# Weight pieces loaded to other places and earlier, x split by ScalarE and GpSimd, and the activation ahead of the mask

## What is computed

```python
def _attn_ref(q, k, v, tau):
    scores = scale * np.matmul(q, k.transpose(0, 1, 3, 2))
    thresh = np.max(scores, axis=-1, keepdims=True) - tau
    scores = np.where(scores >= thresh, scores, -1000000000.0)
    scores = scores - np.max(scores, axis=-1, keepdims=True)
    attn = np.exp(scores)
    attn = attn / (np.sum(attn, axis=-1, keepdims=True) + 1e-09)
    return np.matmul(attn, v)
def _moe_ref(x, w_in, w_out, alpha):        # 512 -> 2048 -> 512
    h = x @ w_in
    return (np.maximum(h, 0.0) + alpha * np.minimum(h, 0.0)) @ w_out
def _moe2_ref(x, w1, w2, w3, w_out):        # 512 -> 1024 -> 512
    return (((x @ w1) * (x @ w2)) @ w3) @ w_out
```

## Time and profile before

| | us |
|---|---|
| median of 3 timed runs | 1059.4 (1058.19 to 1060.02) |
| the profiled execution | 1060.03 |
| its span | 1058.1 |

### The profile page before, as it was taken

The page is one execution under the profiler, slowest core; times in us unless marked ns, Lnnn a source line. Parts: engine busy times, 40 slices in busy tenths (PEclk is TensorE's granted clock), DMA queues, the critical chain, the costliest instruction groups (busy, mean ns, idle before and its releaser), DMA issues.

```text
span 1058.1 us, 18205 instructions
## 1 busy us (share of the span) xinstructions
PE 990.3 (94%) x6848; PEld 899.6 (85%) x6848; DVE 519.6 (49%) x1374; ACT 420.0 (40%) x1000; POOL 472.2 (45%) x580
## 2 busy tenths in 40 slices
PE   3799956999999999999999999999999999999998
PEld 2566634777877787889999999999999999999998
DVE  6888977899998998922332222222111111111111
ACT  5666655666665666434323333333111111211210
POOL 5877768766666656323444444444212111111211
PEclk9799986999999999999999999999999999999999
DMA  7389898787878686768153222263211011011000
GB/s 261 86 242 276 263 302 199 197 229 185 234 196 237 184 208 181 198 168 300 56 198 131 113 112 113 112 250 133 91 68 45 24 68 46 23 68 46 24 23 24
DMA packets 53224, 156.39 MB, mean 148 GB/s; under 512 B 8208, under 2 KB 20496, under 8 KB 49424
## 3 DMA queue, kind: packets, MB, share of 16 engines
q1 hardware_dynamic: 42144, 122.78, 37.3%
q10 hardware_dynamic: 10992, 32.45, 10.8%
HBM read 79.05 MB, written 32.51 MB: 105 GB/s over the span
## 4 chain that ended last, share of the span: by engine, by line
PE 61%; DVE 13%; DMA 7%; POOL 5%; issue 5%; ACT 4%; SPq 4%; ACTq 1%; POOLq 0%
PE psum L693 19%; PE psum L726 19%; PE psum L679 11%; PE psum L638 5%; DVE nmx L940 5%; DMA zbuf<-ybuf 4%; DVE e_ring L953 4%; PE psum L600 3%; SPq L443 3%; POOL g L1069 2%; PE psum L651 2%; PE psum L583 2%; DVE g_raw L985 1%; ACT g_raw L840 1%; DMA k_raw<-k 1%
## 5 line engine op out<-in xcount | busy, mean ns | idle before, releaser
L1069 POOL TENSOR_TENSOR g<-g_raw,g 128x288 fp32r<-128x288 f32 x192 | 158.7, 831 | 378.8 <-ACT g L922 235.1
L726 PE MATMUL psum<-xy,w_a 128*128 128x288 f32 x1536 | 206.1, 295 | 0.6 <-DVE y_buf L1053 0.6
L726 PEld LDWEIGHTS psum<-xy,w_a 128*128 128x128 f32 x1536 | 205.2, 188 | 0.8 <-DVE y_buf L1053 0.8
L583 PE MATMUL psum<-ks,qs 128*128 128x288 f32 x640 | 121.4, 320 | 37.3 <-DVE e_ring L953 25.3
L583 PEld LDWEIGHTS psum<-ks,qs 128*128 128x128 f32 x640 | 101.2, 204 | 53.9 <-DVE e_ring L953 35.5
L1098 POOL TENSOR_SCALAR e_ring<-e_ring,rden,uni 128x576 f32<-128x576 f32 x144 | 118.6, 825 | 60.3 <-DVE rden L964 56.8
L805 ACT ACTIVATE e_ring<-psum,nmx 128x576 f32<-128x576 f32 x144 | 106.7, 741 | 82.1 <-DVE nmx L940 82.0
L985 DVE SCALAR_TENSOR_TENSOR g_raw<-g_raw,beta_sb,psum 128x288 f32<-128x288 f32 x128 | 65.7, 514 | 127.2 <-ACT g_raw L840 127.0
L953 DVE SCALAR_TENSOR_TENSOR e_ring<-psum,thr,e_ring 128x576 f32<-128x576 f32 x144 | 115.4, 801 | 12.4 <-ACT e_ring L805 11.9
L600 PE MATMUL psum<-zbuf,vs 128*64 128x320 f32 (+1 forms) x640 | 107.9, 433 | 13.7 <-DMA zbuf<-ybuf 10.9
L940 DVE TENSOR_REDUCE nmx<-psum 128x1 f32<-128x576 f32 x144 | 108.5, 753 | 22.7 <-PE psum L583 22.3
(11 more groups left out here) (53 smaller groups left out, 1105.7 us busy)
## 6 DMA issues: line engine op xcount, KB each, us to landing
zbuf<-ybuf SPq DMA_DIRECT2D x96, 180.0 KB, 4.4
raw_a<-weights SPq DMA_DIRECT2D x56, 256.0 KB, 6.9
zbuf<-ybuf SPq DMA_DIRECT2D x96, 144.0 KB, 4.3
xy<-xs SPq DMA_DIRECT2D x12, 1152.0 KB, 5.2
q_raw<-q ACTq DMA_DIRECT2D x16, 576.0 KB, 6.2
xs<-x_hl SPq DMA_DIRECT2D x32, 288.0 KB, 6.1
ys<-xy SPq DMA_DIRECT2D x8, 1152.0 KB, 4.4
xy<-ys SPq DMA_DIRECT2D x8, 1152.0 KB, 5.1
```

The lines of the kernel that those rows point to most:

```text
L583: last = mm(dst, qs[:, par, at:at + P], ks[:, par, part, h, cols], start=(m == 0), stop=(m == 2 * len(terms) - 1))
L726: last = mm(psum[:, 2 * ab + f % 2, 0:CH], w_a[:, wp, slot, (f % 4) * P:(f % 4 + 1) * P], xy[c][:, xp, kt, :], start=(n == 0), stop=(n == ...
L1069: sub = lambda out_, a, hi: nc.gpsimd.tensor_tensor(out_, a, hi.bitcast(F32), ALU.subtract)
```

## The change

It has five parts.

1. The eight up weight pieces 24 to 31 ("parked") are loaded in steps 10 to 13, two a step, without a wait: four into the place where the chunk's x (xy_0) will stand, four into the upper part of g. Each has its own semaphore. Their split stays at steps 45 to 55 and now waits for the product on ScalarE. SP waits for the lo parts of pieces 24 to 27 ahead of the first chunk's load, ScalarE for those up to piece 31 ahead of the eighth hi part of g of chunk 0.
2. The split of pieces 32 to 39 moves to steps 58 to 68 by a new list.
3. x leaves PSUM as plain fp32, by ScalarE in four pieces, into the place of its lo part; ScalarE then casts the whole 128x576 from SBUF after the exp of the step of the last two pieces, and GpSimd subtracts in one instruction, after the lo part of an activation. VectorE has no part in it. TensorE waits for the evacuation (s_xe) ahead of the next values product, where it waited for the lo part.
4. Of the ten lo parts of pair 0 VectorE makes six in step 2 and four in step 10, ahead of the mask of tile 0. The loads of the keys and queries of pair 1 are issued in steps 2 and 9, not 4 and 8.
5. VectorE makes a late activation ahead of the mask.

```diff
-PIECE_STEPS += [45, 46, 48, 49, 51, 52, 54, 55, 57, 58, 60, 61, 63, 64, 66, 67]
+PIECE_STEPS += [45, 46, 48, 49, 51, 52, 54, 55, 58, 59, 61, 62, 64, 65, 67, 68]
...
+def parked(k):
+
+    return N_WP <= k < N_WP + FT
...
 def load_step(k):
+    if parked(k):
+        return TILES + 1 + (k - N_WP) // 2
     return 0 if k < 2 * FT else PRODUCT_STEPS[4 * product_before(k) + 3] + 2 + max(0, k - N_WP - FT) // 2
...
+        def raw_piece(j):
+            if not parked(j):
+                return raw_a[:, 1, early_slot(j), :]
+            at = (j - N_WP) % 4 * PC
+            return raw_xy[:, at:at + PC] if j < N_WP + 4 else raw_g[:, 4 * PC + at:4 * PC + at + PC]
...
             def load_piece(j):
 
                 slot = early_slot(j)
+                if parked(j):
+                    sp.dma_start(raw_piece(j), weights[j]).then_inc(s_park[j - N_WP], 16)
+                    return
                 if product_before(j) is not None:
                     sp.wait_ge(s_wp, product_before(j) + 1)
-                sp.dma_start(raw_a[:, 1, slot, :], weights[j]).then_inc(s_w_in[slot], 16)
+                sp.dma_start(raw_piece(j), weights[j]).then_inc(s_w_in[slot], 16)
...
                 if ck >= 1:
                     sp.wait_ge(s_h, FT * ck)
+                else:
+                    sp.wait_ge(s_w_lo[0], N_WP + 4)
...
-                sp.wait_ge(s_xl, X_PARTS * (n + 1))
+                sp.wait_ge(s_xl, n + 1)
...
-                        pe.wait_ge(s_xl, X_PARTS * n - 2 + 2 * y)
+                        pe.wait_ge(s_xe, X_PARTS * n - 2 + 2 * y)
...
             def early_hi(j):
                 slot = early_slot(j)
-                act.wait_ge(s_w_in[slot], 16 * loads_into(j))
-                copy(w_a[:, 0, slot, :], raw_a[:, 1, slot, :]).then_inc(s_w_hi, 1)
+                piece_loaded(act, j)
+                if parked(j):
+                    act.wait_ge(s_wp, product_before(j) + 1)
+                copy(w_a[:, 0, slot, :], raw_piece(j)).then_inc(s_w_hi, 1)
...
-                dst, src = x_piece(n, part)
-                copy(dst[0], src).then_inc(s_xh, 1)
+                copy(*x_piece(n, part)).then_inc(s_xe, 1)
+
+            def x_hi(n):
+                act.wait_ge(s_xe, X_PARTS * (n + 1))
+                copy(x_hl[:, n % 2, 0, :], raw_x[:, n % 2, 1, :]).then_inc(s_xh, 1)
...
                 act.wait_ge(s_g, FT * cc + (f + 1))
+                if (cc, f) == (0, FT - 1):
+                    act.wait_ge(s_w_lo[0], N_WP + FT)
...
                 if tile_at(s) is not None:
                     exp_of(tile_at(s))
+                if pair_at(s, LAG_X[1]) is not None:
+                    x_hi(pair_at(s, LAG_X[1]))
...
-                if s % TILES == 4 and s // TILES + 1 < NPAIR:
+                if s == 2:
+                    load_keys(1)
+                elif s % TILES == 4 and TILES < s < TILES * (NPAIR - 1):
                     load_keys(s // TILES + 1)
-                if s % TILES == 8 and s // TILES + 1 < NPAIR:
+                if s == LEAD:
+                    load_queries(1)
+                elif s % TILES == 8 and TILES < s < TILES * (NPAIR - 1):
                     load_queries(s // TILES + 1)
...
+                if s == LEAD + 1:
+                    for low in FIRST_LO[FIRST_KEYS:]:
+                        first_lo(low)
+                for ck, f in hidden_late(s - 1):
+                    activation_of(ck, f, 0, fbank(f))
                 if tile_at(s, 1) is not None:
                     mask_of(tile_at(s, 1))
-                for ck, f in hidden_late(s - 1):
-                    activation_of(ck, f, 0, fbank(f))
...
-                for part in range(X_PARTS):
-                    if pair_at(s, LAG_X[part // 2]) is not None:
-                        x_lo(pair_at(s, LAG_X[part // 2]), part)
...
+            def x_lo(n):
+                pool.wait_ge(s_xh, n + 1)
+                sub(x_hl[:, n % 2, 1, :], raw_x[:, n % 2, 1, :], x_hl[:, n % 2, 0, :]).then_inc(s_xl, 1)
...
                 for ck, f in hidden_done(s - 1):
                     activation_lo(ck, f)
+                if pair_at(s, LAG_X[1]) is not None:
+                    x_lo(pair_at(s, LAG_X[1]))
```

41 lines of the change are left out of this document (25 added, 16 removed).

## The result

The changed kernel takes 1079.3 us (median of four runs, 1076.7 to 1085.1) where the kernel before takes 1059.7 us (four runs, 1058.2 to 1064.7): 1.0184 times the time, 95% interval 1.013 to 1.0238. It is slower; whether by more or less than 2% the interval leaves open. It is also 8 us slower than forecast. Of all the executions behind this document one, of a_mask_first, took 2409.9 us; its ratio leaves it out.

A forecast was written before the change was run, and what follows sets the result against it. Until 444 us the loop of max, exp, relu, activation was taken to bound the kernel, then TensorE. 16.7 - 2.8 - 1.0 - 1.5 + 0.6 + 0 = +12.0 us gave 1071.4 us; range from 1055, with a little room, to 1080.

The forecast's parts named there:

- a loop cost of 25 us: Upper bound for five chunks: six late activations a chunk each cost a full 0.73 us, plus 0.58 us.
- The activation ahead of the mask: Chunks beside tiles: the mask enters the max, exp, relu, activation loop; 3.34 us per chunk, +16.7 us over five.
- The step at position 3: Fourth of a chunk's 18 steps, counted from 0: 3.51 us grows to 4.46 us, +0.95.
- position 9: Chunk step of f7's activation: delayed mask holds up scores, +0.55 us, with +0.38 handed on from positions 6 and 8.
- Rival A: TensorE has enough queued work at positions 2 to 9 to hide the longer loop; 1055 us, chance 0.20.
- x split: VectorE loses 1.24 us of subtractions per pair: -2.8 us in the chunks, -1.0 us in steps 28 to 57.
- The half at position 9: VectorE's saved 0.6 us at positions 0 and 9 gains nothing, as TensorE or the relu ends the wait.
- the half at position 11: Of positions 2 and 11, the saving counts at 11 alone, where TensorE later waits for ScalarE's copy: -2.8 us.
- Up weights early: ScalarE's weight-piece stall near 150 us goes; 4.0 us gained at 148.9 shrink to -1.5 us at 178.
- First pair: Front: tile 0's 3.8 us lead is lost, a late query load is won back by tile 9; 0 us.
- + 0.6: Chunk 0, position 4: a later down weight piece's 0.6 us cast stands ahead of the relu.
- Rival B: VectorE's own work sets the steps, so each pair's 1.24 us counts in full; 1044 us, chance 0.08.

The follow-up runs named there:

- a_mask_first: The changed kernel with the mask put back ahead of the late activation; 1061.5 us, ratio 1.0007 to the kernel before.
- b_act_first: The kernel before with only VectorE's late activation moved ahead of the mask; 1075.9 us, ratio 1.0146.
- b_x_split: The kernel before with only the split of x by ScalarE and GpSimd; 1061.6 us, ratio 1.001.
- b_parked: The kernel before with only the up weights loaded early and the new steps of the down pieces; 1057.7 us, ratio 0.9987.
- b_first: The kernel before with only four first lo parts after the first max and the second pair's loads at steps 2 and 9; 1059.4 us, ratio 1.0006.
- p_late_down: b_parked with the down pieces loaded in steps 59 to 62 and split at 64 to 71; 1055.4 us, ratio 0.9966 to the kernel before.
- p_relu_x: p_relu_first with x split by ScalarE and GpSimd; 1051.8 us, ratio 0.9913 to the kernel before.
- p_relu_first: p_late_down with ScalarE's late relus at the end of their own step, ahead of key and query casts; 1050.4 us, ratio 0.9896 to the kernel before.
- a_hold_y: a_mask_first with each chunk's second and third output stores issued later, at position 17; 1061.8 us, ratio 1.0035 to the kernel before.
- p_keys_later: p_relu_x with the key loads from pair 3 on issued two steps later; 1045.5 us, ratio 0.9864 to the kernel before.
- p_relu_act: p_relu_first with the late activation ahead of the mask; 1059.1 us, ratio 1.0 to the kernel before.

## Why the prediction was right, and where it fell short

The direction and the reason hold; the time lies inside the range, at its upper end, 8 us above the forecast of 1071.4. That the range held is in part luck: its upper end was drawn for a loop cost of 25 us, the loop cost 19, and a term that is not in the sum at all filled the room.

*The activation ahead of the mask* (+16.7) was right in place and size. The step at position 3 was forecast at 4.46 us and is 4.45; its increment over the typical chunks is 0.94 (0.95 forecast), position 2 has 0.75 (0.73), position 9 0.74 (0.55, and 0.38 that came from 6 and 8; these showed 0.16 and 0.23 of their own, 0.39). Position 4 has 0.97, not 0.73. Together 3.8 us a chunk, 19 over five, where 3.34 and 16.7 were forecast; alone the order costs 15.5 us, undone from the whole 17.8. Rival A, that TensorE hides it, would have b_act_first within 0.2% of the kernel before; it is 1.46% slower.

*x split* (-2.8 in the loop, -1.0 ahead of it): the gain is there and larger, and it is eaten. The half at position 9, to which I gave nothing, is worth 0.46 us, seen at position 10, and the half at position 11 is worth 0.71 us, seen at 12: 5.9 us over five chunks, twice the 2.8 by which I bounded it. Ahead of the chunks, too, it is more than the 1.0 forecast: the steps of tiles 22, 31, 40 and 49 are 0.65 to 0.72 us shorter, and what takes that back is the stall ahead of tile 44. **The step that failed is a term that I didn't have**: I set the new wait of TensorE for the evacuation and the later store of x at nothing, and never asked when the next pair's blocks land and when a shorter loop asks for them.'s stretch has 0.6 us of such waits, and a list of waits doesn't show slack: in the trace of before the last move landed 0.34, 0.27 and 0.18 us ahead of TensorE's asking for pairs 6, 8 and 12, and 0.57 us behind it for pair 10. The price is 12.7 us of longer first steps in one trace of the changed kernel and 7.4 in the other, 11.4 in b_x_split; b_parked and b_first, without the new split, have 2.9 each, so some 3 us of such a sum can come without it. To this come the 4.6 us ahead of tile 44 (3.6 in the second trace).

*Up weights early* (-1.5): the first half was exact, 148.30 against 148.9 for the max behind the stall, and so was the warning that the gain shrinks in the full DMA queues: tile 55 is at -0.1. I was also wrong about where it would stand: TensorE's wait that ended at 178.57 is gone, and one of 10.35 us stands at tile 53 in front of the first half of the same blocks. It needs the early weights and the split of x together (b_parked 2.99 us, b_x_split 3.80), a meeting of two parts that I had priced one by one; p_late_down and p_relu_x, where it is gone, suggest that it needs the down weights in the way as well. The Trainium skill's rule that each DMA engine alternates between queues at packet granularity (DMA: Bandwidth & Descriptors, "Queues, rings and completion order") is no comfort for this. The trace agrees with it: of SP's moves issued behind ScalarE's key load of 156.85 three landed before it and the others after it, so neither queue stood behind the whole of the other. But the key load took 15.5 us where it took 9.2. SP's own moves were issued behind SP's weights and the chunk's x, and the median of the larger ones rose from 5.6 to 12.9 us.

*First pair*: 0 forecast, 0 measured (b_first 1.0006). The late query load is there: its first cast stands at 24.86 us, forecast near 24.3, and tile 4 is 1.54 us late; tile 9 starts at 38.44, as before. Tile 1 shows why the lead of 3.6 us at tile 0 is gone, ScalarE's wait for the second pair's keys until 16.54. The timeline of the changed kernel:

```profile
10.11 0.76 DVE L987 TENSOR_REDUCE nmx<-psum 128x1 f32<-128x576 f32 x1 [0.62 <-PE psum L613]
...
15.62 0.75 DVE L987 TENSOR_REDUCE nmx<-psum 128x1 f32<-128x576 f32 x1
...
16.54 0.67 ACT L804 CAST ks<-k_raw 128x576 fp32r<-128x576 f32 x1 [3.88 <-DMA k_raw<-k]
...
24.86 0.60 ACT L804 CAST qs<-q_raw 128x512 fp32r<-128x512 f32 x1
```

*The sum.* Inside the chunks I forecast 16.7 - 2.8 + 0.6 = +14.5 and the balance shows +13.0, two errors (loop too small, x too small) that cancel. Before step 64 I forecast -2.5 and it shows -0.1 and +3.6 in the two traces. The term that isn't in my sum, the blocks at the chunks' first steps, is +12.7 and +7.4. The medians ask for 19.6 us in all.

Rival B (VectorE's own work sets the steps) had the kernel at 1044 us. It fell with the loop positions of b_x_split, of which 2 and 9 are no shorter and 10 and 12 alone gain, and with p_relu_first, which changes no engine's work but only ScalarE's order and is 5 us faster than p_late_down. The Trainium skill's way of finding the contended engine by its busy share (Perfetto Trace Analysis, "Identifying the Most-Contended Engine") would have led to B here: neither engine was at its limit, the loop through three of them was. At positions 10 and 12 B is right even so: there VectorE's work does set the step, as the 0.46 and 0.71 us show, and most of what it gains is lost to the blocks.

**What stays open.** What of the longer first steps is TensorE asking sooner and what is the blocks landing later, since the second differs from trace to trace by as much as it changes. The output stores have at most a small part in it (a_hold_y). The load of the keys among the moves has one: at tile 44 its place ahead of SP's last move makes the stall, and p_keys_later removes it. Why ScalarE reaches that load some 0.6 us sooner with the new split, and x's store on SP, now issued later, were not tested by themselves; nor was the meeting of the early weights with the split of x alone. And it is open why the same program's moves land differently from trace to trace.

## What to carry to other kernels

In an engine that runs in order, an operation that sits in front of a wait is free as far as it fits into that wait; moved behind the wait it costs up to its full length in each turn of the loop (here 0.73 of 0.80 us at positions 2 and 9, and 0.16 to 0.37 at 3, 6 and 8), so read the order around each wait before moving anything, and move the operation that others wait for (here the relu, 5 us) ahead of those that nobody needs yet. Before a loop is shortened, compare for every transfer that it consumes the moment it lands with the moment it is asked for: the list of waits shows only slack that is already gone. A large load that is issued from another queue just ahead of a move that is waited for can cost more than the whole gain (here 0.6 us sooner, and 2 to 5 us lost at tile 44), so look at the order of issues over both queues. And a stall that is removed while the stretch behind it stays full can come back at the next transfer: two weight groups out of the stretch gave 3.6 us, one gave 1.4, within the noise.

## What the runs showed of the hardware

The instructions on the engines repeat from trace to trace: of the 143 steps from max to max 113 are equal to 0.015 us in the changed kernel's two traces. The transfers don't repeat: in two traces of the same program the last of 16 block moves of the same pairs landed 18.3, 19.2, 20.0 and 20.2 us, and 17.3, 17.9, 18.7 and 20.0 us, after the first was issued. The start of tile 55 differed by 3.7 us between these two traces. Nearly all of it came at tile 19, with the DMA engines full (share 0.99 and 1.03 from 55 to 70 us): in one trace TensorE waits 2.2 us there for pair 0's blocks, and the step is 3.5 us longer. The same step is 4.5 to 6.0 us longer than before in three other traces (a_mask_first, p_relu_first, p_relu_act) and at most 1.3 us in the remaining nine. From the kernel before to b_first and b_act_first, which load the same things from 144 us on, tile 55 differs by 3.8 and 0.9 us. A gain of a few us at a DMA-bound stall can't be read from one trace.

The granted clock adds to such a stall. In the stretch with the idle 10 us it was 0.57 of full speed (0.73 before), near the lower of the two levels, 1.2 GHz; from 190 to 475 us, with TensorE waiting more than before, it was 0.98 (1.00 before, 190 to 450 us) and from 480 us on 1.00. The eight value matmuls behind the stall at 171.97 took 2.37 us, the same eight at 263.25 took 1.29. The windows of the changed kernel (start:end, length, each engine, clock, DMA share, GB/s):

```profile
190.00:475.00 285.00, 253.23 (x1688) 207.49 (x1689) 230.20 (x648) 165.03 (x389) 176.03 (x226) 0.98 0.72 188
...
152.00:180.00 28.00, 13.83 (x55) 9.04 (x55) 17.02 (x50) 12.73 (x28) 18.82 (x22) 0.57 1.02 229
480.00:1080.00 600.00, 596.74 (x4440) 589.96 (x4439) 123.37 (x240) 147.36 (x377) 176.30 (x202) 1.00 0.26 96
```
